# The experts' first layer as seven block products of 384 columns for eight

## The reference

```
p = domain_probs / (domain_probs.sum(-1, keepdims=True) + 1e-09)
for e in range(4):
    h = np.maximum(x @ w1[e], 0.0)          # 1536 x 320 @ 320 x 1024
    out += p[:, e:e + 1] * (h @ w2[e])      # 1536 x 1024 @ 1024 x 320
```

## Time and profile before

| | us |
|---|---|
| three runs | 583.67, 584.20, 584.64 (median 584.2) |
| span of the profiled execution, first to last instruction | 582.2 |
| TensorE busy (matmuls) | 578.0 |
| VectorE, ScalarE, GpSimd busy | 222.7, 201.2, 128.4 |

### The profile page before, as it was taken

The page is one execution under the profiler, slowest core; times in us unless marked ns, Lnnn a source line. Parts: engine busy times, 40 slices in busy tenths (PEclk is TensorE's granted clock), DMA queues, the critical chain, the costliest instruction groups (busy, mean ns, idle before and its releaser), DMA issues.

```text
span 582.2 us, 8993 instructions
## 1 busy us (share of the span) xinstructions
PE 578.0 (99%) x3668; PEld 527.4 (91%) x3668; DVE 222.7 (38%) x451; ACT 201.2 (35%) x399; POOL 128.4 (22%) x102
## 2 busy tenths in 40 slices
PE   9999999999999999999999999999999999999997
PEld 8999999999998888899999999999999999999997
DVE  6656656565565333313131313131323232222222
ACT  5775655565434555411123211123211111111111
POOL 4987333332200444400004300014200000000000
PEclk9999999999999999999999999999999999999999
DMA  7987845563210223300003200001000000001011
GB/s 270 342 288 245 304 105 166 169 169 97 52 40 0 86 98 103 111 2 1 0 1 100 99 1 0 1 1 50 2 1 1 1 1 0 1 0 46 1 45 46
DMA packets 39054, 44.33 MB, mean 76 GB/s; under 512 B 21190, under 2 KB 31686, under 8 KB 39014
## 3 DMA queue, kind: packets, MB, share of 16 engines
q1 hardware_dynamic: 38912, 43.71, 23.5%
q10 hardware_dynamic: 102, 0.05, 0.0%
HBM read 39.02 MB, written 4.73 MB: 75 GB/s over the span
## 4 chain that ended last, share of the span: by engine, by line
PE 99%; DVE 0%; issue 0%; ACT 0%; DVEq 0%
PE bank L1359 11%; PE bank L1358 11%; PE bank L1360 11%; PE bank L1417 10%; PE bank L1416 10%; PE bank L1415 10%; PE bank L1361 6%; PE bank L1365 5%; PE bank L1387 5%; PE bank L1388 4%; PE bank L1389 4%; PE bank L1147 2%; PE bank L1396 2%; PE bank L1395 2%; PE bank L1198 1%; PE bank L1169 1%
## 5 line engine op out<-in xcount | busy, mean ns | idle before, releaser
L1112 DVE SCALAR_TENSOR_TENSOR g_lo<-bank,g_hi 128x512 fp32r<-128x512 f32 x96 | 66.3, 691 | 253.5 <-ACT g_hi L827 253.5
L827 ACT ACTIVATE g_hi<-bank 128x512 fp32r<-128x512 f32 x96 | 57.5, 599 | 269.8 <-PE bank L1365 269.7
L1417 PE MATMUL bank<-w_all,g_lo 128*128 128x320 f32 x384 | 118.7, 309 | 0.0
L1416 PE MATMUL bank<-w_all,g_hi 128*128 128x320 f32 x384 | 118.5, 309 | 0.0
L1359 PE MATMUL bank<-x_lo,w_all 128*128 128x512 f32 (+2 forms) x318 | 118.2, 372 | 0.0
L1415 PE MATMUL bank<-w_all,g_hi 128*128 128x320 f32 x384 | 118.2, 308 | 0.0
L1358 PE MATMUL bank<-x_hi,w_all 128*128 128x512 f32 (+2 forms) x318 | 117.9, 371 | 0.0
L1360 PE MATMUL bank<-x_hi,w_all 128*128 128x512 f32 (+2 forms) x318 | 117.0, 368 | 0.0
L613 POOL TENSOR_TENSOR w_all<-w_raw,w_all 128x1408 fp32r<-128x1408 f32 x16 | 51.7, 3230 | 192.5 <-ACT w_all L702 192.5
L1415 PEld LDWEIGHTS bank<-w_all,g_hi 128*128 128x128 f32 x384 | 72.1, 188 | 3.7
L1416 PEld LDWEIGHTS bank<-w_all,g_hi 128*128 128x128 f32 x384 | 72.1, 188 | 3.7
(11 more groups left out here) (165 smaller groups left out, 656.6 us busy)
## 6 DMA issues: line engine op xcount, KB each, us to landing
w_raw<-in_w SPq DMA_DIRECT2D x24, 704.0 KB, 4.3
zb<-z SPq DMA_DIRECT2D x10, 512.0 KB, 5.3
feat<-in_feat SPq DMA_DIRECT2D x10, 512.0 KB, 4.2
tok<-in_tok SPq DMA_DIRECT2D x10, 484.0 KB, 5.2
spare<-xg SPq DMA_DIRECT2D x8, 256.0 KB, 2.8
out<-arena SPq DMA_DIRECT2D x12, 160.0 KB, 1.9
fb<-f SPq DMA_DIRECT2D x16, 80.0 KB
xg<-feat SPq DMA_DIRECT2D x16, 80.0 KB
```

Source lines behind the costliest of these rows:

```text
L827: A(g_hi[:, b, 0:N], h_ps[b][:, 0:N], ACT.Relu).then_inc(ghi_ready, 1)
L1112: V.scalar_tensor_tensor(g_lo[:, b, 0:N], h_ps[b][:, 0:N], 0.0, g_hi[:, b, 0:N].bitcast(F32), ALU.max, ALU.subtract).then_inc(g_ready, 1)
L1416: mm(out, g_hi[:, b, t], low_w, start=False, stop=False)
L1417: last = mm(out, g_lo[:, b, t], high_w, start=False, stop=stop)
```

## The change

**Blocks.** For each expert the first layer is cut in two along the 320 features (160 = 128 + a tail of 32), in two along a pair of hidden tiles, and in two along 768 tokens, a half of all (`WIDE` = 384). Strassen's form (Winograd's) gives the four result blocks C11, C12, C21, C22 from seven block products where the plain way has eight. It needs sums of weight blocks (S1 to S4) and of x blocks (T1 to T4). A block product is four matmuls of 384 columns: high*high, high*low, low*high, and one of 96 rows in which the tail's three pairs stand above each other.

**Units.** The experts' 96 steps become 32 units `u` (4 experts x 2 halves x 4 pairs). Products 1 and 2 collect in one bank (C11), 7 and 4 in a second, 5 and 3 in the first again, 6 in the second before. ScalarE copies product 1 to SBUF, VectorE makes U2 = P1 + P6, U3 = U2 + P7, C22 = U3 + P5, C21 = U3 + (P7's bank gives P4), C12 = U2 + (P5's bank gives P3) in SBUF. Each C block is rounded by ScalarE (`high_tile`) and its rest taken by VectorE (`low_tile`), for C11 from the bank, for the others from SBUF. Twelve second-layer parts (`third`, three matmuls of 320 columns as before) of the unit before stand between the products. After four units VectorE's six mixes stand in three places of the next unit.

**Weights and x.** GpSimd makes S1 to S4 (`add_weights`), T1 to T4 (`add_x`) and the weights' rests (`low_weights`); ScalarE and VectorE round and take rests of seven x blocks for each half. The new buffers lie over old ones. SP copies x's tails to four places (`spread_tails`) and loads a piece with four DMAs (`load_fast`), into a ring of two. A piece's weights serve two units; ScalarE rounds them in the units 1, 6 to 9, 14 to 17 and 22 to 25 (`fast_at`), the first three pieces still in the first MLP. In unit 0 the products' order is 1, 6, 7, 5, 2, 4, 3, and the first MLP's last `down_rows` stands behind product 1.

The diff, cut to what the text speaks of:

```diff
+            def load_fast(q):
+                ...
+                    sp.wait_ge(fast_down, q - FAST_RING + 1)
+                sp.dma_start(fast_raw[:, r, 0:RAW_TAIL], w_d[k, :, 0:RAW_TAIL]).then_inc(fast_in[r], 16)
+                for half in range(2):
+                    ...
+                    sp.dma_start(fast_raw[:, r, c:c + UPW], rows).then_inc(fast_in[r], 16)
+                sp.dma_start(fast_raw[:, r, RAW_DN:RAW_PIECE], w_d[k, :, DN0:PIECE]).then_inc(fast_in[r], 16)
+            def spread_tails(h):
+                sp.wait_ge(xt_ready, 3 + h)
+                for half in range(2):
+                    for r in range(4):
+                        sp.dma_start(x2[32 * r:32 * r + 32, 3 + half, c], x2[32 * half:32 * half + 32, 2, c])\
+                          .then_inc(tails_in, 16)
 # GpSimd
-            for k in range(WARM, PIECES):
-                split_low(k)
+            def add_weights(q):
+                pool.wait_ge(fast_in[q % FAST_RING], 64 * (q // FAST_RING + 1))
+                G.tensor_tensor(second, raw_block(q, 1), raw_block(q, A22), ALU.add).then_inc(sums_of_w, 1)
+                ...
+                pool.wait_ge(sums_of_w, 4 * q + 3)
+                G.tensor_tensor(fourth, raw_block(q, A12), third, ALU.subtract).then_inc(sums_of_w, 1)
+            def low_weights(q):
+                pool.wait_ge(sums_of_w, 4 * q + 4)
+                for part, (c, n, src) in enumerate(((0, 4 * P, raw[:, 0:RAW_DN].rearrange("p (m c) -> p m c", m=2)),
+                                                    (4 * P, 3 * P, w_sums[:, :, :]))):
+                    pool.wait_ge(high_up, 2 * q + part + 1)
+                    G.tensor_tensor(w[:, F_LOW + c:F_LOW + c + n], src[:, 0, :], w[:, c:c + n].bitcast(F32),
+                                    ALU.subtract).then_inc(fast_low, 1)
+                    ...
+                    G.tensor_tensor(tail_, src[32:64, 1, :], tail_.bitcast(F32), ALU.subtract).then_inc(fast_up, 1)
+                    ...
+                pool.wait_ge(high_down, q + 1)
+                G.tensor_tensor(w[:, F_DN + 2 * D:F_PIECE], raw[:, RAW_DN:RAW_PIECE], w[:, F_DN:F_DN + 2 * D].bitcast(F32),
+                                ALU.subtract).then_inc(fast_down, 1)
+            def add_x(h):
+                pool.wait_ge(x2_main, 6 + 2 * h)
+                pool.wait_ge(tails_in, 128 * (h + 1))
+                ...
+                    G.tensor_tensor(x_sum(h, i), one, two_, ALU.subtract).then_inc(x_sums, 1)
 # ScalarE
+            for u in range(E_UNITS):
+                first_product(u)
+                if u in fast_at:
+                    q = fast_at[u]
+                    high_weights(q, 0)
+                    high_weights(q, 1)
+                    high_of_down(q)
+                ...
+                act.wait_ge(product_made, made(u, 2))
+                high_tile(u, C11, bank_of(u, 2)[:, 0:WIDE])
+                act.wait_ge(summed, 5 * u + SUM_C22)
+                high_tile(u, C22, sum_b)
+                act.wait_ge(summed, 5 * u + SUM_C21)
+                high_tile(u, C21, sum_c)
+                act.wait_ge(summed, 5 * u + SUM_C12)
+                high_tile(u, C12, half_sums[:, u % 2, :])
 # VectorE
+            def low_tile(u, k, src):
+                dve.wait_ge(tile_high, 4 * u + k + 1)
+                V.scalar_tensor_tensor(g_tiles[:, k, 1, :], src, 0.0, g_tiles[:, k, 0, :].bitcast(F32),
+                                       ALU.max, ALU.subtract).then_inc(tile_low, 1)
+            def add_product(u, name, out, other):
+                dve.wait_ge(product_made, made(u, name))
+                V.tensor_tensor(out, bank_of(u, name)[:, 0:WIDE], other, ALU.add).then_inc(summed, 1)
+            for u in range(E_UNITS):
+                sum_a = half_sums[:, u % 2, :]
+                add_product(u, 6, sum_a, sum_a)
+                ...
+                if u:
+                    low_tile(u, C11, bank_of(u, 2)[:, 0:WIDE])
+                    ...
+                add_product(u, 7, sum_b, sum_a)
+                add_product(u, 5, sum_b, sum_b)
+                low_tile(u, C22, sum_b)
+                if u > PPU - 1 and u % PPU == 0:
+                    for tt in range(TPB):
+                        mix(u // PPU - 1, tt)
+                add_product(u, 4, sum_c, sum_a)
+                low_tile(u, C21, sum_c)
+                if u > PPU - 1 and u % PPU == 0:
+                    for tt in range(TPB, TPH - 1):
+                        mix(u // PPU - 1, tt)
+                add_product(u, 3, sum_a, sum_a)
+                low_tile(u, C12, sum_a)
+                ...
+                if u > PPU - 1 and u % PPU == 0:
+                    mix(u // PPU - 1, TPH - 1)
 # TensorE
+            product(0, 1)
+            down_rows(L1_STEPS - 1)
+            ...
+            for u in range(1, E_UNITS):
+                pe.wait_ge(summed, 5 * (u - 1) + SUM_C21)
+                product(u, 1)
+                third(u - 1, 0)
+                third(u - 1, 1)
+                pe.wait_ge(summed, 5 * (u - 1) + SUM_C12)
+                product(u, 6)
+                third(u - 1, 2)
+                third(u - 1, 3)
+                pe.wait_ge(first_copied, u + 1)
+                product(u, 2)
+                third(u - 1, 4)
+                third(u - 1, 5)
+                pe.wait_ge(summed, 5 * u + SUM_U2)
+                product(u, 7)
+                third(u - 1, 6)
+                third(u - 1, 7)
+                pe.wait_ge(tile_low, 4 * u + C11 + 1)
+                product(u, 5)
+                third(u - 1, 8)
+                third(u - 1, 9)
+                pe.wait_ge(summed, 5 * u + SUM_U3)
+                product(u, 4)
+                third(u - 1, 10)
+                pe.wait_ge(summed, 5 * u + SUM_C22)
+                product(u, 3)
+                third(u - 1, 11)
+            for t in range(12):
+                third(E_UNITS - 1, t)
```

More of the change, by code:

```diff
@@ L66 @@
 GRP = 4 * CH
[L67 to L70, removed]
 WARM = 2 * PPU
-PIECES = UNITS * PPU
+HALVES = 2
+HALF = TOK // HALVES
+WIDE = HALF // 2
+TPB = WIDE // P
+TPH = 2 * TPB
+FAST = EXPERTS * PPU
+E_UNITS = EXPERTS * HALVES * PPU
+A11, S3, A12, A22, S1, S2, S4 = range(7)
+B11, B21, B22, T1, T2, T3, T4 = range(7)
+BLOCKS = 7
+PRODUCTS = {1: (A11, B11), 2: (A12, B21), 3: (S4, B22), 4: (A22, T4), 5: (S1, T1), 6: (S2, T2), 7: (S3, T3)}
+KT = 96
+TILES = ((0, 0), (1, 1), (1, 0), (0, 1))
+C11, C22, C21, C12 = range(4)
+SUM_U2, SUM_U3, SUM_C22, SUM_C21, SUM_C12 = range(1, 6)
+F_TAIL = BLOCKS * P
+F_LOW = 2 * BLOCKS * P
+F_DN = 3 * BLOCKS * P
+F_PIECE = F_DN + 4 * D
+RAW_TAIL = 4 * P
+RAW_DN = 8 * P
+RAW_PIECE = RAW_DN + 2 * D
+FAST_RING = 2
 WARM_UP = 4
@@ L357, in tile_of @@
         def tile_of(m):
[L359 to L370, removed]
@@ L830, in _ @@
[L830 to L832 removed]
+                after(act, g_ready, m - 1)
+                A(g_tmp[:, b, 0:N], h_ps[b][:, 0:N], ACT.Tanh).then_inc(tanh_done, 1)
+                if m == 0:
+                    act.wait_ge(wv_ready, BATCH)
+                    A(wa[:, :, :], bank[4][:, 0:3 * ROWS].rearrange("p (k r) -> p k r", r=ROWS),
+                      ACT.Copy).then_inc(wa_ready, 1)
@@ new lines, in _ @@
+                for n, k in phase(m):
+                    if turns(n, k) and not by_feature(n):
+                        x_high(n, c_ps)
+                    if turns(n, k) and by_feature(n) and n < STEPS - 1:
+                        x_high_feat(n)
+                    if k == 1:
+                        gate(n)
+                for k in range(2, WARM):
+                    if split_at[k] == m - 1:
+                        split_rest(k)
+                act.wait_ge(h_less, m + 1)
+                after(act, down_done, m - 1)
@@ L1124, in _ @@
+            for tt in range(TPH):
+                mix(EXPERTS * HALVES - 1, tt)
         @block.tensor
@@ L1429, in _, with new_half @@
+            def new_half(u, j):
+                if u % (2 * PPU) == PPU and u < 2 * PPU:
+                    pe.wait_ge(block_ready, BLOCKS + j + 1)
+            for m in range(L1_STEPS):
                 up(m)
```

550 lines of the change are left out of this document (337 added, 213 removed).

## The result

The changed kernel takes **593.9 us** in the median (593.63 to 594.3, four runs); the kernel before, on the same chip, 584.4 (583.67 to 584.95). The ratio is 1.016, 95% interval 1.0145 to 1.0174. It is slower by 9.4 us, where 582.5 was forecast. The profiled span is 591.8 us at a granted clock of 1.00, 9.6 us above the span before, so the loss lies in the span and can be looked for in the trace. One execution of the whole study, the profiled one of "second layer first alone", took 1944.8 us; it is left out of that run's median, and no row of it is shown.

What follows compares the result with a forecast made beforehand. TensorE's instruction stream was taken as the bound, busy 99% of 582.2 us. 582.2 - 19.1 + 0.6 + 1.0 + 0.3 + 12.1 + 3.4 = 580.5 of span, plus 2.0 carried over: 582.5 us; range 575 to 590.

Steps and rivals of the forecast that it cites:

- Matmuls removed: TensorE, experts' first layer: 768 matmuls of 512 columns become 896 of 384, units of 10.18 us, saving 19.1 us.
- The handover: From first MLP to experts: only product 1 covers the chain to g before the last second-layer step, +0.6 us.
- unit 0: First experts' unit, without second-layer parts to fill waits: product 1 of unit 1 waits for a VectorE sum, +1.0 us.
- the hold: VectorE instructions lengthened where GpSimd works at the same time; forecast 0.64 us on a unit's chain, 0.5 in unit 0.
- A plain unit waits for nothing: Units without mixes or pieces: VectorE's sums reach products 1 and 6 with 0.66 and 0.64 us to spare.
- Units that mix: Seven units whose mixes stand ahead of VectorE's adds of products 4 and 3: 1.73 us each, +12.1 us.
- Weights, x blocks, DMAs: Extra preparation on SP, GpSimd, ScalarE and VectorE runs ahead of TensorE: counted 0, at most 1 us.
- GpSimd and VectorE: Experts' units: VectorE's rests from SBUF lose time meeting GpSimd's instructions, +3.4 us, between 0 and 10.
- The prediction's own sign: Waits of TensorE before product 5 or 2 would make the forecast's VectorE chain wrong.
- Rival 2: GpSimd's round of 11.7 us against units of 10.18 becomes the bound, delaying C11 and product 5: 589.5 us, chance 0.28.
- The chance of 0.33 for slower: Chance given to a measured time above the kernel before by more than 1.2 us, summed over forecast and rivals.

Runs made afterwards that it cites:

- second layer first alone: Changed kernel with only the second layer's copy and rest moved ahead of those of the blocks, from piece 4 on: 585.3 us.
- the mixes apart: Changed kernel with the six mixes of a mixing unit spread out in VectorE's order, all work done: 580.9 us.
- the writes: Two runs of the changed kernel, GpSimd's sums and rests from piece 4 on replaced by memsets; four writes for the sums 583.9 us, five 589.4 us.
- the run with four writes: Changed kernel with GpSimd's sums and rests from piece 4 on replaced by memsets, four of them for the sums: 583.9 us.
- the run with the sums of x behind the first rests: Mixes apart, second layer first, x-block rests moved, plus GpSimd's first-MLP x sums waiting for VectorE's rests of B11, B21, B22: 578.0 us.

## Why the prediction was wrong

- **Matmuls removed (-19.1): right.** The unit is 10.18 us, and 96 rows turn like 128.
- **The handover (+0.6) and unit 0 (+1.0): right or a little high**, 8.23 for 8.31, and the 0.5 for the hold in unit 0 did not come.
- **A plain unit waits for nothing: right** in units 11, 19, 27, 30. Unit 11 has the slack too: the add of product 4 ends at 363.59, a restart stands 0.05 behind an add (286.26 + 0.55 to 286.86), and product 1 starts at 364.31: 0.67 for 0.66.
- **Units that mix (+12.1): right**, 12.5, in the mechanism and in the two waits.
- **Weights, x blocks, DMAs ("I count 0, at most 1 us"): wrong**, +1.9, of which 1.7 lie between 190 and 200 us. The step looked at the DMAs ahead of the first block and at the engines' sums of work, and not at VectorE's rests beside GpSimd's sums of x, though the next step knew that such pairs exclude each other.
- **GpSimd and VectorE (+3.4): the step that failed.** It charged a mean hold of 0.64 in the first unit of each group (1.9) and nothing in the others, and left the round of 11.7 us, worked out from rows under the second rival, out of the forecast. The groups lost 9.9: 1.7 to 2.0 of each 3.35 come with such a round alone, the others with the holds. The mean over phases met at random was wrong as well: the three groups lose 3.36, 3.35 and 3.20, so the meetings repeat from group to group. In units 1 to 3 the forecast had 1.0, nothing and 0.3, and they lost 0.09, 1.93 and 0.89: the place was wrong, and the sum less wrong than its parts. The prediction's own sign said so: it had named waits before product 5 as proof against its chain, and they stand in units 2, 8, 16 and 24.
- **Rival 2** had the mechanism, the place (C11 behind ScalarE's wait, product 5) and the size of a group (2 us above the hold's 0.64; measured 3.35 in all), and gave 589.5. It had 1 us for the x blocks, and they cost 1.9 + 1.6: with that it comes to 592. Against it I had set that four units without pieces follow, and that each mix stall gives the round 1.7 us. The four units do give it back, but not before the third and fourth piece are late. The stalls didn't help: with the mixes apart a group still loses 3.2 us, no more than with them (3.35). The bound it named, 10.6, is near what the writes show: 10.77 costs 0.1 us a group, 11.57 costs 1.7 to 2.0.

The chance of 0.33 for slower was too small, and for a reason that could be seen: each term of rival 2 had a row, and neither argument against it was worked out piece by piece.

## What to carry to other kernels

For each new instruction on a side engine, ask what stands behind it and who waits for that, not how busy the engine is: five mixes of 0.5 us on a VectorE at 57% cost 1.8 us in one place and nothing in another. Where an engine prepares a part for each turn of the main one, compare its full round, its waits for other engines in, with the turn; what it can do while it waits is found in its own list of work. When a saving on the main engine (19 us here) is bought with a chain over three side engines, give that chain's slack a number first: here 0.66 us decided what the mixes and the holds cost.

## What was not expected of the hardware

- A matmul that restarts TensorE after a wait of 0.4 to 1 us takes a turn of 0.25 to 0.29 in place of 0.175 (287.14 - 286.86), and the printed wait is shorter than the delay. The list shows 17.6 us of waits in the experts' stage, where the units from 1 on have 12.5 + 9.9 + 2.9 = 25.3 us beyond 10.18.
- An instruction of GpSimd that only writes doesn't hold VectorE: the rests from SBUF take 571 ns on the mean in the run with four writes and 696 in the kernel after (over 96 rests, most of which meet nothing). (The Trainium skill, SBUF — State Buffer, Who interferes with whom, says that a VectorE instruction with two SBUF inputs contends with a GpSimd instruction that reads SBUF, not with one that only writes it. The trace agrees, and also with its rule that one input from a bank is free of it: 557 ns in both kernels.)
- After 3.75 us without work for TensorE the granted clock was at half (1.2 for 2.4 GHz) from some point behind the restart at 220.74 to about 225, with TensorE at work all the time. In the run with the sums of x behind the first rests, the columns being us, busy time of five engines, granted clock, DMA share and GB/s:

```profile
217.00:221.00 4.00, 0.26 (x1) 0.26 (x2) 1.71 (x3) 3.18 (x5) 2.59 (x3) 1.00 0.32 103
221.00:223.00 2.00, 2.00 (x7) 1.58 (x7) 1.34 (x3) 1.24 (x3) 1.92 (x2) 0.64 0.00 0
223.00:225.00 2.00, 2.00 (x6) 1.52 (x6) 0.27 (x1) 0.28 (x1) 1.92 (x3) 0.51 0.00 0
225.00:227.00 2.00, 2.00 (x10) 1.65 (x9) 0.06 (x1) 0.60 (x1) 1.91 (x3) 1.00 0.46 132
```
